# Earlier waits for the state's decay on GpSimd, and another order at the end of a tile

## What is computed

```python
# 1. a linear recurrence, per batch b (4), head h (8), 48 x 48 complex state, 768 steps
new_re = ar * S_re - ai * S_im ; new_im = ar * S_im + ai * S_re
S_re, S_im = new_re + outer(k[t], v[t]), new_im
y[t] = q[t] @ S_re                      # a_re, a_im are first limited to magnitude 0.999
# 2. a dense layer on the 3072 rows y (384 wide)
h = x @ w_in                            # 384 x 1024
e = exp(h - max(h)); solu = h * e / sum(e)
x2 = ((solu - mean) / sqrt(var + 1e-6) * g_ln) @ w_out    # 1024 x 384
# 3. a mixture of 8 experts, two for each row
noisy = x2 @ w_gate + log1p(exp(x2 @ w_noise)) * noise    # the best two columns pick the experts
out[row] += weight * (relu(x2[row] @ w1[e]) @ w2[e])
```

## Time and profile before

| | us |
|---|---|
| median of 3 runs | 1214.07 (1211.77 to 1214.28) |
| the profiled execution | 1212.83 |
| its span, first to last instruction | 1211.1 |
| first phase | to about 653 |
| TensorE busy over the span | 1041.4 (86%) |
| VectorE, ScalarE, GpSimd busy | 872.8, 621.1, 449.7 |
| mean granted clock of TensorE | 0.944 of full speed |

### The profile page before, as it was taken

The page is one execution under the profiler, slowest core; times in us unless marked ns, Lnnn a source line. Parts: engine busy times, 40 slices in busy tenths (PEclk is TensorE's granted clock), DMA queues, the critical chain, the costliest instruction groups (busy, mean ns, idle before and its releaser), DMA issues.

```text
span 1211.1 us, 21883 instructions
## 1 busy us (share of the span) xinstructions
PE 1041.4 (86%) x7866; PEld 984.5 (81%) x7866; DVE 872.8 (72%) x1729; ACT 621.1 (51%) x967; POOL 449.7 (37%) x417
## 2 busy tenths in 40 slices
PE   0046988988998998899964999999999999999996
PEld 0035887877887887788864999999999999999996
DVE  6888779879969969945553777667676767776672
ACT  6432663764664664544532555555555555555551
POOL 4110241252352352243523244345434533543442
PEclk9977998998898898899986999999999999999998
DMA  9420220230230210211404666767676767676640
GB/s 231 174 76 27 54 86 27 67 86 27 66 87 27 64 37 27 58 42 53 125 14 156 227 233 226 253 234 256 202 267 235 253 227 244 228 230 235 209 162 1
DMA packets 85980, 167.51 MB, mean 138 GB/s; under 512 B 18566, under 2 KB 57696, under 8 KB 85872
## 3 DMA queue, kind: packets, MB, share of 16 engines
q1 hardware_dynamic: 72432, 137.71, 36.1%
q0 software_dynamic: 13440, 28.40, 6.4%
HBM read 148.83 MB, written 21.92 MB: 141 GB/s over the span
## 4 chain that ended last, share of the span: by engine, by line
PE 55%; issue 2%; ACT 1%; DVE 1%; DMA 1%; POOL 0%; POOLq 0%; DVEq 0%; ACTq 0%; SPq 0%
PE bank L1367 22%; PE bank L1547 21%; PE bank L1411 3%; PE bank L1358 3%; PE bank L1459 3%; PE bank L1433 1%; PE bank L1491 1%; PE bank L1471 0%; ACT z L859 0%; DMA xg<-xs,mine 0%; PE bank L1477 0%; PE bank L1387 0%; DMA tags<-tag,idx 0%; ACT x L856 0%; ACT x2t L867 0%
## 5 line engine op out<-in xcount | busy, mean ns | idle before, releaser
L899 ACT ACTIVATE hh<-bank 128x256 fp32r<-128x256 f32 x248 | 95.3, 384 | 256.6 <-PE bank L1367 256.6
L1367 PE MATMUL bank<-sxh,w1h 128*128 128x256 f32 x744 | 212.1, 285 | 2.1 <-DVE sxl L1317 2.1
L1367 PE MATMUL bank<-sxh,w1l 128*128 128x256 f32 x744 | 210.3, 283 | 0.0
L1367 PE MATMUL bank<-sxl,w1h 128*128 128x256 f32 x744 | 210.0, 282 | 0.0
L1336 DVE SCALAR_TENSOR_TENSOR hl<-bank,hh 128x256 fp32r<-128x256 f32 x248 | 104.8, 423 | 120.8 <-ACT hh L899 109.0
L672 POOL DMA_INDIRECT out<-yo,mine x62 | 77.9, 1256 | 277.8 <-DVE yo L1329 268.4
L1547 PE MATMUL bank<-w2h,hh 128*128 128x384 f32 x496 | 167.4, 337 | 0.0
L1547 PE MATMUL bank<-w2l,hh 128*128 128x384 f32 x496 | 166.8, 336 | 0.0
L1547 PE MATMUL bank<-w2h,hl 128*128 128x384 f32 x496 | 166.6, 336 | 0.0
L1367 PEld LDWEIGHTS bank<-sxh,w1h 128*128 128x128 f32 x744 | 140.8, 189 | 2.5 <-DVE sxl L1317 2.5
L1367 PEld LDWEIGHTS bank<-sxh,w1l 128*128 128x128 f32 x744 | 141.5, 190 | 0.0
(11 more groups left out here) (184 smaller groups left out, 2353.4 us busy)
## 6 DMA issues: line engine op xcount, KB each, us to landing
raw<-in_w SPq DMA_DIRECT2D x62, 1536.0 KB
ar<-in_a_re SPq DMA_DIRECT2D x6, 768.0 KB, 4.7
turn<-in_a_im SPq DMA_DIRECT2D x6, 768.0 KB, 7.0
qk<-in_q SPq DMA_DIRECT2D x48, 96.0 KB, 2.4
qk<-in_k SPq DMA_DIRECT2D x48, 96.0 KB, 2.5
out<-wide SPq DMA_DIRECT2D x9, 512.0 KB, 11.3
vt<-in_v SPq DMA_DIRECT2D x24, 192.0 KB, 2.6
xs<-x SPq DMA_DIRECT2D x24, 192.0 KB, 2.7
```

The source lines that it names most:

```text
L899: nc.scalar.activation(hh[:, f % NH, :], bank[:, f % 2, 0:CAP], ACT.Relu).then_inc(hh_done, 1)
L1367: ins = MM(dst, stationary[a_](cc), moving[b_](cc), start=(n_ == 0), stop=(n_ == len(terms) - 1))
```

## The change

`decay_state` is cut in its three instructions. In body n GpSimd now starts with step 0, which also waits for `zt_hi` (ScalarE's zh of tile n-3 is written, so VectorE can begin zl); step 1 waits for `h_mm` (the matmuls with w_in are done, so VectorE can begin nmax); step 2 waits for `exp_done` (the exp is done). Step 0 stands ahead of `m2(2c+3)`, step 2 ahead of the masking of at.

The end of a tile is in another order. On ScalarE x2t comes ahead of the centring, and the square behind xh; its output is a new tile `squared` in SBUF. In body 3 `inverse(2c+2)` comes ahead of x2t. On VectorE the state's sum follows at once on the softmax (six fills and f2 stood between), ten fills stand between kp and xl, and the rest of the body's fills behind qp (all stood ahead of xl). TensorE's L1411 waits for VectorE's solu rather than for the square before it overwrites banks 4 and 5.

```diff
+    def decay_state(t, step):   # step 0: waits w_added, m_step, md_spread, state_step, then st2
...                              # step 1: st3; step 2: waits state_step, then state
+                if decays:
+                    pool.wait_ge(zt_hi, min(n - 2, T))
+                    decay_state(n, 0)
                 if b == 0 and prep and c > 0:
                     m2(2 * c + 3)
+                if decays:
+                    pool.wait_ge(h_mm, min(i + 1, T))
+                    decay_state(n, 1)
+                    pool.wait_ge(exp_done, min(i + 1, T))
+                    decay_state(n, 2)
                 if has(m):
...
-                if B <= n < T:
-                    decay_state(n)
...
+                if b == 3 and prep:
+                    inverse(2 * c + 2)
                 if has(j):
...
+                    nc.scalar.activation(squared[:], z[:], ACT.Square, accum_out=mv[i % 2][:, 2:3]).then_inc(var_done, 1)
...
-                fill(6)
-                if b == 3 and prep:
-                    f2(2 * c + 2)
-                    f2(2 * c + 3)
                 if 0 <= m < LIVE:
...
-                fill(share - made[0])
+                fill(10)
                 if has(m):
                     dve.wait_ge(xt_hi, m + 1)
...
+                fill(share - made[0])
...
-                    wait(pe, var_done, i)
+                    wait(pe, solu_step, 4 * i)
```

More of the change, by code:

```diff
@@ L160, in solu_moe_program @@
         mhalf = m1("mhalf", [P, 2])
+        squared = m1("squared", [P, F])
         g_sb = m1("g_sb", [P, FC])
@@ L606, in body @@
                 prep = c + 1 < C
+                decays = B <= n < T
+                if decays:
+                    pool.wait_ge(zt_hi, min(n - 2, T))
+                    decay_state(n, 0)
                 if b == 0 and prep and c > 0:
                     m2(2 * c + 3)
+                if decays:
[3 more added lines that the diff above has]
+                    decay_state(n, 2)
                 if has(m):
@@ L867, in body @@
                     nc.scalar.activation(x2t[:].rearrange("p c t -> p (c t)"), bank[:, 3, 0:DM], ACT.Copy).then_inc(x2t_evac, 1)
-                if b == 3 and prep:
-                    inverse(2 * c + 2)
+                if has(i):
+                    act.wait_ge(solu_step, 4 * i + 4)
+                    nc.scalar.activation(z[:], z[:], ACT.Identity, bias=mv[i % 2][:, 1:2]).then_inc(centred, 1)
                 if has(m):
@@ L1259, in body @@
                                     bank[:, 6, 0:2 * NP * D], ALU.add).then_inc(w_added, 1)
+                if b == 3 and prep:
+                    f2(2 * c + 2)
+                    f2(2 * c + 3)
                 if has(n):
```

32 lines of the change are left out of this document (15 added, 17 removed).

## The result

The changed kernel takes 1222.3 us, median of 5 runs (1219.8 to 1225.4), beside 1211.8 us for the kernel before on the same chip (5 runs): ratio 1.0092, 95% interval 1.0070 to 1.0113. It is 0.9% slower. The forecast was 1219 us, slower, 0.4% over the median then known. The profiled execution took 1225.4 us, its span is 1223.6 us against 1211.1, so there are 12.5 us between the traces to account for. zl is VectorE's instruction L1199 (L1209 after), one in each body. From the last zl of the first phase to the end it is 588.3 us, 589.3 before, so the loss is ahead of that.

What follows compares the result with a forecast made beforehand. First phase decides; neither TensorE (82 of 92 us a chunk) nor VectorE (79) alone bounds it, TensorE's waits being VectorE's. 13.3 - 1.6 - 3.3 - 2.6 - 0.7 = 5.1 us slower: 1219 us, own range 1216 to 1223, 8 in 10 1208 to 1228.

Steps and rivals of the forecast that it cites:

- the stall: Body 0, chunks 1 to 4: step 0 waits for md, delaying m2 and ScalarE's second logs; 13.3 us lost.
- chunk 0: First chunk, without decays: xl ahead of more fills lets L1411 begin earlier; 3.3 us gained once.
- the rival of the clock: TensorE runs at 1.2 GHz after standing still ahead of L1411 in bodies 2 and 3: 6 us more, 1225 us, chance 0.20.
- Bodies 1 to 3: VectorE beside GpSimd's steps there: 0.4 us gained in each of four chunks, 1.6 us together.
- My ledger of meetings: VectorE instructions slowed beside GpSimd, per chunk: 6.1 us lost before, 8 or 9 meetings costing 5 to 6 after.
- The place of xl: VectorE's xl ahead of four fills in body 1, three in body 2: worth nothing in chunks 1 to 4.
- Chunk 5 and the drain: End of first phase: 0.7 us gained in chunk 5's body 0, 2.6 us once in the drain from earlier x2t.
- Free steps: Rival: steps 0 and 1 cost nothing in bodies 2 and 3 either, 9.6 us less; 1210 us, chance 0.16.
- The half absorbed stall: Rival: in body 0 md is through earlier, a chunk loses 2.0 us rather than 3.3; 1213 us, chance 0.14.
- The square into SBUF: ScalarE's square written to SBUF: 0 to 0.12 us more for each of 24, taken as none in the sum.

Runs made afterwards that it cites:

- E4: Changed kernel with the decay back at its old place on GpSimd, three steps in a row without the waits, new order kept: 1205.6 us, ratio 0.9947.
- E5: Changed kernel with only body 0's decay back at its old place without waits; waits stay in bodies 1 to 3: 1202.9 us, ratio 0.9943.
- E2: Changed kernel with SyncE issuing the six DMAs of md ahead of the six of cum: 1209.2 us, ratio 0.9971.
- E6: Changed kernel with 24 more identity transposes on TensorE in its gap in body 0 of chunks 1 to 4: 1219.1 us, ratio 1.0075.
- E1: Changed kernel with m2(2c+3) moved ahead of step 0 of the decay on GpSimd, nothing else: 1214.0 us, ratio 1.0012.
- E8: E4 with all fills ahead of xl on VectorE: 1211.8 us, ratio 1.0028.
- E12: E10 plus only VectorE's part of the change, the other engines keeping E10's order: 1188.0 us, ratio 0.9811.
- E10: Kernel before with one edit, ScalarE's second scale of chunks 1 to 4 behind zh of body 1: 1200.8 us, ratio 0.9907.

## Why the prediction was right, and where it was not

The direction was right, for the reason given. The size was less than half of what came: 0.4% forecast, 0.9% measured, and +5.1 us in the sum against +12.5 in the ledger. Two terms lie outside their own bounds, the stall (16.9 us, bounds 11.7 to 16.1) and chunk 0 (4.6, bounds 1.5 to 3.6), and 1222.3 us is nearer to the rival of the clock (1225) than to the forecast (1219); what sets the two apart are the traces and experiments, not the time.

**The direction and its cause held.** Step 0 of the decay ahead of m2 makes ScalarE's second logs wait for the landing of md, and nothing hides it. E4 and E5 take the stall away by putting the decay of body 0 back, E2 by letting md land earlier, and each ends below the kernel before.

**The stall's term** was 16.1 less 2.8 given back, 13.3; the trace shows 17.0 us of wait and 16.9 in the ledger. The wait was sized well, by one DMA's issue and landing. The 0.7 given back in each chunk did not come: from L867 to zl it is 10.3 us in chunk 4 (445.76 to 456.03), as before (10.2). I named the square, which the change put last and on which rstd and the second zsum depend, and still laid out a gain from the earlier x2t and transposes. With the clock kept up it comes in one of the three chunks in which E6 fills the gap. E1 splits the 16.9: 9.1 are m2's place in the queue, 7.8 what is left with m2 first: the mask, the zsum, the tags and rstd behind a wait for md. Of the 7.8, E2 leaves 1.4 in place, so that up to 1.4 may have another cause.

**Bodies 1 to 3** were to gain 1.6 and lose 3.7. The mechanism was right, the size of the term not. The md computation came out clean but for its last instruction, step 1 can fall on nmax, and steps 0 and 1 push out fills in body 2, as the prediction put it. My ledger of meetings had these weigh less than what is saved. E5, where no stall disturbs, has -1.2, +4.8 and -2.4 against before, +1.2 in all: 0.3 lost a chunk where I had 0.4 gained. The other 2.5 of the changed kernel are these: "1 to 2" gains nothing, and in two of four chunks (2 and 4) hidden in body 2 runs longer at 1.2 GHz, 8.6 and 8.7 us against 7.2 and 7.3, and the interval to the next mark is 25.4 and 25.5 against 24.1. That is not the stall's alone: E5, without it, has one such chunk (8.2 us for hidden, 25.1 for the interval), E1 three and E2 none.

**The place of xl** was "worth nothing in chunks 1 to 4". E8 shows 5.7 us for it in "2 to 3" alone. The step "VectorE comes to the next nmax no earlier" failed: with hidden later, nmax waits for it, 4.2 us in all, so VectorE had no such lag. It stayed unseen in the sum, because the rest of the order costs about as much: before and E4 have the same chunks 1 to 4 (341.6 and 341.9), while E8, with that rest alone, has 348.3. Two errors of 6 us with opposite signs hid each other; that this term of the sum came out near nothing was luck.

**Chunk 0** gave 4.6 where I had 3.3. Of these xl's place is 3.1 (E8); 1.4 is the other order, on VectorE as well, since E12 has all of it (4.9 less than E10). **Chunk 5 and the drain** gave 3.5; I had 3.3 (2.6 and 0.7). In the drain x2t now comes 1.2 us after x rather than 4.0, and the next x 14.6 us after this one rather than 16.8: 2.2 of the 2.6.

**The rivals.** Free steps (1210 us): E5 against E4 says that the steps are worth nothing measurable; it falls. The half absorbed stall (1213 us) falls: nothing is absorbed. The clock (1225 us): its gaps are there (2.9 us ahead of hidden in body 2, 3.4 in body 3 of chunk 4), and by the longer hidden and the longer intervals of two chunks it adds some 2.6 us (1.3 each), less than half of what I gave it. That is read from the traces; no run fills these gaps, so it is not shown. The rest of the +6.1 in "2 to 3" is there in E5 too, whose hidden in body 2 takes as long as E4's (7.3 us in three chunks of four), so it is not the clock's.

**The sum**, term by term, in us:

| term | predicted | ledger |
|---|---|---|
| chunk 0 | -3.3 | -4.6 |
| body 0, stall | +13.3 | +16.9 |
| bodies 1 to 3 | -1.6 | +3.7 |
| chunk 5 and drain | -3.3 | -3.5 |
| sum | +5.1 | +12.5 |

The chunks from 141 us on take 95.7, 98.1 and 96.7 us (the first three), where the prediction had about 95.

**The square into SBUF** takes 1.056 us a piece, 1.028 into PSUM before (15 and 16 of them from 141 to 509 us). That is 0.03 us each. The Trainium skill (ScalarE: Activation LUTs, Step-by-step: what each stage is for) says that PSUM is the faster destination for ScalarE; by that rule, the trace agrees in sign, with a size that does not matter.

## What to carry to other kernels

When an instruction is moved up on an in-order engine and it has a wait for a DMA, price all that is queued behind it, not the first one alone: here m2 was 9 of 17 us, and the mask, the zsum, the tags and rstd were most of the rest. Before building waits that aim one engine's work at another's free moments, look at what waits at the end of the same bodies: a scale that could stand behind zh, and an xl that stood behind fills nobody waited for, were worth 1.9%, the aimed waits nothing. And before calling a low clock the cause, run the same gap filled with work, and look at each chunk whether the filler covered it.
